# Downsampled attention scores: four half-array matmuls in two PSUM banks instead of three with a block-diagonal operand

## What is computed

```python
q_d = q.reshape(B, H, Sd, factor, D).mean(axis=3)     # Sd = 144, factor = 4, D = 64
k_d, v_d = ...                                        # the same
out_d = sm_attn(q_d, k_d, v_d)                        # 144 x 144 scores for each head
out_up = np.repeat(out_d, factor, axis=2)
...                                                   # local attention, |i - j| < 4
x = (out_up + out_local) as (B*S, H*D)
x = leaky_relu(x @ w_in1) @ w_out1                    # d_model 512, d_ff 2048
x = h - tanh(h), h = x @ w_in2; x @ w_out2
```

## Time and profile before

| what | value |
|---|---|
| median of three runs | 989.72 us (986.1 to 992.62) |
| the profiled execution, its own time | 990.84 us |
| its span, first to last instruction | 989.1 us |
| TensorE's granted clock, mean over the span | 0.984 of full speed |
| busy, share of the span | TensorE 97%, DVE 59%, ACT 56%, POOL 42% |

### The profile page before, as it was taken

How to read it: one execution, slowest core, us unless ns; L and a number is a source line. 1 busy time by engine, 2 the same in 40 slices (tenths; PEclk the granted TensorE clock), 3 DMA queues, 4 the chain that set the end, 5 groups by cost and what they waited for, 6 DMA issues and landing times.

```text
span 989.1 us, 19759 instructions
## 1 busy us (share of the span) xinstructions
PE 956.0 (97%) x6960; PEld 892.1 (90%) x6960; DVE 579.4 (59%) x1066; ACT 554.5 (56%) x1355; POOL 411.5 (42%) x341
## 2 busy tenths in 40 slices
PE   6789999999999999999999999999999999999998
PEld 5678999999999999999999988889899899898996
DVE  5745653664556446635324766776676676766764
ACT  4445644544635446446354767775575666766654
POOL 4535732723616417227161837623233233233232
PEclk9769999999999999999999999999999999999999
DMA  7842421022112211210100302100000000000000
GB/s 168 179 138 66 112 50 35 16 49 49 25 24 49 49 25 24 49 27 10 55 1 30 110 24 76 42 33 1 1 32 1 32 0 0 32 0 0 32 1 32
DMA packets 87797, 41.48 MB, mean 42 GB/s; under 512 B 60352, under 2 KB 81344, under 8 KB 87744
## 3 DMA queue, kind: packets, MB, share of 16 engines
q1 hardware_dynamic: 87744, 40.78, 15.7%
HBM read 36.04 MB, written 4.72 MB: 41 GB/s over the span
## 4 chain that ended last, share of the span: by engine, by line
PE 78%; ACT 6%; DVE 6%; POOL 5%; issue 3%; DMA 2%; SPq 0%; ACTq 0%; POOLq 0%; DVEq 0%
PE ph L474 12%; PE ph L476 11%; PE ph L475 11%; PE acc L550 6%; PE acc L551 6%; PE acc L552 6%; PE acc L503 6%; PE acc L504 5%; PE acc L505 5%; PE banks L372 3%; PE banks L404 2%; DVE g_lo L872 2%; POOL pl L993 2%; PE banks L391 2%; POOL g_lo L1039 1%
## 5 line engine op out<-in xcount | busy, mean ns | idle before, releaser
L1039 POOL TENSOR_TENSOR g_lo<-scratch,g_hi 128x384 fp32r<-128x384 f32 x96 | 126.1, 1314 | 259.3 <-ACT g_hi L664 259.3
L887 DVE TENSOR_TENSOR g<-g,ph 128x288 f32<-128x288 f32 x128 | 57.9, 452 | 189.4 <-ACT g L684 188.5
L1009 POOL TENSOR_TENSOR in_lo<-w_whole,in_hi 128x512 fp32r<-128x512 f32 x64 | 83.8, 1310 | 160.9 <-ACT in_hi L648 159.7
L474 PE MATMUL ph<-x_hi,w_hi_a 128*128 128x288 f32 (+1 forms) x448 | 144.7, 323 | 1.9 <-DVE x_lo L867 1.9
L684 ACT ACTIVATE g<-ph 128x288 f32<-128x288 f32 x128 | 52.5, 410 | 157.2 <-PE ph L476 155.8
L476 PE MATMUL ph<-x_hi,w_lo_a 128*128 128x288 f32 (+1 forms) x448 | 140.5, 314 | 0.0
L475 PE MATMUL ph<-x_lo,w_hi_a 128*128 128x288 f32 (+1 forms) x448 | 140.4, 313 | 0.0
L923 DVE SCALAR_TENSOR_TENSOR scratch<-scratch,ph 128x384 f32<-128x384 f32 x96 | 53.2, 554 | 112.9 <-ACT scratch L729 108.0
L1014 POOL TENSOR_TENSOR out_lo<-w_whole,out_hi 128x512 fp32r<-128x512 f32 x64 | 86.4, 1350 | 56.3 <-ACT out_hi L652 55.6
L728 ACT ACTIVATE scratch<-ph 128x384 f32<-128x384 f32 x96 | 46.8, 488 | 108.4 <-PE ph L476 106.8
L872 DVE TENSOR_TENSOR g_lo<-g,g_hi 128x288 fp32r<-128x288 f32 x128 | 88.6, 692 | 2.7 <-ACT g_hi L664 2.7
(11 more groups left out here) (162 smaller groups left out, 2688.8 us busy)
## 6 DMA issues: line engine op xcount, KB each, us to landing
out_dram<-o_stage SPq DMA_DIRECT2D x18, 256.0 KB, 2.0
w_whole<-in_moe_w_in_dram SPq DMA_DIRECT2D x16, 256.0 KB, 3.6
w_whole<-in_moe_w_out_dram SPq DMA_DIRECT2D x16, 256.0 KB, 4.4
qn<-in_q_dram SPq DMA_DIRECT2D x28, 144.0 KB
kn<-in_k_dram SPq DMA_DIRECT2D x28, 144.0 KB
v4n<-in_v_dram SPq DMA_DIRECT2D x28, 144.0 KB
vw<-in_v_dram SPq DMA_DIRECT2D x28, 122.5 KB
scratch<-in_moe_w_in_dram SPq DMA_DIRECT2D x8, 256.0 KB, 2.9
```

Of the source, the lines that this page charges most:

```text
L474: pe.matmul(bank, whi, x_hi[:, c, 0:width], start=(c == 0), stop=False)
L1009: pool.tensor_tensor(in_lo[:, f % 2, :], w_whole[:, f - KEPT, 0:DM], in_hi[:, f % 2, :].bitcast(F32), ALU.subtract).then_inc(in_lo_done, 1)
L1039: pool.tensor_tensor(g2_lo[:, f % 3, :], g2[:, f % 2, :], g2_hi[:, f % 3, :].bitcast(F32), ALU.subtract).then_inc(g_lo_done, 1)
```

## The change

The block-diagonal operand goes. q is summed into `qdT`, 144 columns with both heads in their own rows, by one DVE instruction. Step 6 has four matmuls instead of three: two groups of 72 queries for each of two heads, each on 64 rows of the array; head 0's scores go to bank 0, head 1's to bank 1. So step 6 waits for bank 1 as well, and step 11 waits for bank 0 (the exponentials) where it waited for bank 1. The coarse probabilities have 72 partitions and four groups of 144 instead of 96 partitions and three groups, in the maximum, the exponentials, the scaling and the turns. The order of the engines' lists is unchanged.

```diff
-    QT = 3
+    QT = 4
...
-                self.qd_diag, self.kdT = place("qd_diag", [P, NB, 2, QM]), place("kdT", [P, SD_])
+                self.qdT, self.kdT = place("qdT", [P, SD_]), place("kdT", [P, SD_])
...
             def values_d(s, bank):
-                probs = s.pdT.rearrange("p g (n h m) -> p g n h m", n=NB, h=2)
...
-                                         probs[:, g, :, h, :], start=(g == 0), stop=(g == 1))
+                                         s.pdT[:, g, h * SD_:(h + 1) * SD_], start=(g == 0), stop=(g == 1))
...
                 elif step == 6:
                     pe.wait_ge(s.means_done, 2 * i + 2)
                     pe.wait_ge(s.bank_free[0], uses0(i, 3))
-                    for t in range(QT):
-                        last = pe.matmul(s.banks[0:QP, 0, t * SD_:(t + 1) * SD_],
-                                         s.qd_diag[:, 3 * t:3 * t + 3, :, :].rearrange("p n h m -> p (n h m)"),
-                                         s.kdT[:, :], start=True, stop=True)
+                    pe.wait_ge(s.bank_free[1], uses1(i, 3))
+                    for t in range(QT // 2):
+                        for h in range(2):
+                            rows = slice(h * D, (h + 1) * D)
+                            last = pe.matmul(s.banks[0:QP, h, t * SD_:(t + 1) * SD_], s.qdT[rows, t * QP:(t + 1) * QP],
+                                             s.kdT[rows, :], start=True, stop=True)
                     last.then_inc(s.bank_full[0], 1)
                 elif step == 11:
                     pe.wait_ge(s.norm_l, i + 1)
-                    pe.wait_ge(s.bank_free[1], uses1(i, 3))
+                    pe.wait_ge(s.bank_free[0], uses0(i, 4))
...
                     for t in range(QT):
-                        last = act.activation(s.pd[:, t, :], s.banks[0:QP, 0, t * SD_:(t + 1) * SD_], ACT.Exp,
+                        h, at = divmod(t * SD_, 2 * SD_)
+                        last = act.activation(s.pd[:, t, :], s.banks[0:QP, h, at:at + SD_], ACT.Exp,
...
-                    for h in range(2):
-                        rows = slice(h * D, (h + 1) * D)
-                        last = dve.tensor_reduce(s.qd_diag[rows, :, h, :],
-                                                 s.qT[rows, :].rearrange("p (n m f) -> p n m f", n=NB, f=FACTOR),
-                                                 AX_X, ALU.add)
-                    last.then_inc(s.means_done, 1)
+                    dve.tensor_reduce(s.qdT[:, :], s.qT[:, :].rearrange("p (m f) -> p m f", f=FACTOR), AX_X, ALU.add)\
+                        .then_inc(s.means_done, 1)
...
-                    quarter = s.banks[0:QP, 0, 0:QT * SD_].rearrange("p (t k) -> p t k", t=QT)
-                    dve.tensor_reduce(s.mxd[:, :], quarter, AX_X, ALU.max, negate=True).then_inc(s.max_d, 1)
+                    quarter = s.banks[0:QP, 0:2, 0:2 * SD_].rearrange("p h (t k) -> p h t k", t=2)
+                    dve.tensor_reduce(s.mxd[:, :].rearrange("p (h t) -> p h t", h=2), quarter, AX_X, ALU.max,
+                                      negate=True).then_inc(s.max_d, 1)
...
-                dve.memset(s.qd_diag[:, :, :, :], 0.0)
```

More of the change, by code:

```diff
@@ L113, in two_scale_attention_and_feed_forward @@
         in_xT = {"pT": 0, "vd": 0, "kdT": 0, "up": 0, "qT": 1, "pd": 1, "mxl": 1, "mxd": 1, "rs": 1,
-                 "vw": 2, "qd_diag": 2, "v4n": 3, "pl": 3}
+                 "vw": 2, "qdT": 2, "v4n": 3, "pl": 3}
         taken = [S] * CD
```

## The result

| what | before | after |
|---|---|---|
| median of four runs each | 988.95 us (986.1 to 992.62) | 1001.19 us (998.72 to 1002.86) |
| ratio, 95% interval | | 1.011 (1.0082 to 1.0139) |
| the profiled execution, its own time | 990.84 us | 1002.86 us |
| its span | 989.1 us | 1001.1 us |
| mean granted clock | 0.984 | 0.988 |

The kernel before has one run more here than in the table ahead of the prediction. The forecast was +0.7% and within 1%; it came out at +1.1%, inside the range of 990.0 to 1002.5. The second stage went as forecast. The first stage did not: it lost 7.4 us in the profiled execution (the slowest of the four) and some 3 to 5 us by the timed runs, where 0.8 was forecast.

What follows compares the result with a forecast made beforehand. TensorE, busy 97% of the span, was taken as the bound. Second pairs 5.7, first pairs 0.1 and first stage 0.8 summed to +6.6 us: 996.3 us against 989.72, range 990 to 1002.5.

Steps and rivals of the forecast that it cites:

- The halves overlap: Step 6 on TensorE: matmuls on different row halves run fully side by side, last start 0.37 us after the first.
- The rival without overlap: Step 6: row halves run one after the other, last start 0.85 us after the first; 1001.8 us in all, chance 0.15.
- Entry: Change of array shape going into step 6: 0.23 us instead of 0.13, so +0.10 us a pair.
- Exit: From step 6's last record to the second matmul behind it: 0.45 us instead of 0.25, +0.20 us a pair.
- Net without a wait: Step 6 a pair: entry +0.10, block -0.24, exit +0.20, together +0.06 us; bound without overlap +0.54.
- D: TensorE's lateness after step 6 in second pairs: wait for bank 1 0.63, block -0.24, exit +0.20, together 0.59 us.
- Four exponentials: ACT's exponentials up to the weight split: 0.36 us more than three, 1.45 us in all.
- The rival that they swallow it: Second pairs: ACT and POOL catch up, only D's excess over the L391 stall counts, 0.17 us each; 991.5 us, chance 0.13.
- A second pair: L391 in the second stage's second pairs comes 0.95 us later: 0.59 plus 0.36; six pairs make 5.7 us.
- The rival "faster": DVE's halved L816 brings L829 forward, the wait vanishes and L391's stalls close: -5 us, 985 us; chance 0.04.
- The first stage. ... Together 0.8 us.: First stage: 0.7 us for exponentials on the chain, 0.1 us for step 6 of the first pair; together 0.8 us.
- The 0.7 for the exponentials: First stage, B pair: the fourth exponential stands before the copy L628 that TensorE needs, twice 0.36 us.

Runs made afterwards that it cites:

- e1_wait_only: The kernel before with only the new wait for bank 1 in front of step 6; 3.4 us slower in all.
- e2_exp4_only: The kernel before with a fourth exponential that repeats the last group into spare columns; 2.8 us slower in all.
- e4_filled: The changed kernel with three unused 128x128 matmuls ahead of step 6 of the first B pair; 998.26 us, ratio 1.0076 to the kernel before.
- f12_after_filled: The changed kernel with unused filler matmuls ahead of steps of the first stage and at its end; 996.08 us, ratio 1.0062 to the kernel before.
- f9: The changed kernel with bank 1 freed early on DVE and round 10's weight split listed ahead of the second pair's exponentials on ScalarE; 1012.74 us.

## Why the prediction was right, and where it was not

**Right, with sizes (forecast, measured):**
- The halves overlap. Last record's start 0.37, 0.43 us after the first; the two records of a pair of halves start 7 ns apart. The rival without overlap wanted 0.85: fell.
- Entry 0.23, 0.22 to 0.23. Exit from the last record to the second matmul behind 0.45, 254.23 - 253.78 = 0.45. Net without a wait +0.06, +0.11.
- The wait for L827 hits all second pairs and no first pair but the first stage's. D 0.59, 1.58 - 1.00 = 0.58. That the two agree so well is in part luck: step 6 started 0.05 us after L827's end and not 0.13, and its last record came 0.43 us after the first and not 0.37.
- Four exponentials 1.45, 1.44; L838 0.75, 0.75; no row of TensorE's waits in the changed kernel names POOL's longer scaling of `pd`.
- The stalls swallow nothing in second pairs: the one at L391 grew by 0.36 (0.26 to 0.62). The rival that they swallow it fell. It held for the wait alone: in `e1_wait_only` 0.24 was absorbed. In first pairs 0.10 went into the stall, as argued.
- A second pair +0.95, +1.0; six of them 5.7, 6.
- The halved L816 moved nothing: L827 still ends 0.65 us after L506 starts, where L829 ended 0.64 after L505. The rival "faster" fell, for the reason given, DVE's idle time behind it.

**The step that failed: "The first stage. ... Together 0.8 us."** It measured 7.4 us in the profiled execution. In the timed runs the whole difference is 9.1 to 10.9 us (0.0092 and 0.011 of 990); less 6 for the tiles, that leaves 3 to 5, or 4 to 6 if the 1.3 us that the profiles gain in the second layer stand in the timed runs too, which was not measured. The 0.7 for the exponentials was too high rather than too low: `e2_exp4_only` lost 0.36 us there. Two things were missed. First, the new wait was priced at step 6 of the first A pair alone, where it measured 0.46 us (13.81 against 13.35) for the 0.36 of the sum. At the B pairs it was put at nothing, without a reason. At the first of them the inversion of the A pair (L852, L854) stands between the sum of k and L827, and POOL holds it, so TensorE was 1.14 us more idle (1.42 against 0.28); at the second it stood 1.10 us, where the kernel before did not stand. Secondly, and much larger, the clock was taken as given. The sum used the lower clock for what step 6 itself costs and never asked what a longer stand does to the clock of the work behind it. The rows were there: the clock in that stage was not the full one, so its TensorE work could still take up to twice its time or come back from it. The Trainium skill, TensorE: Matmul & The Clock Gate, Part 1: The HAM clock gate, says that its clock is set by how busy it has been recently; `e4_filled`, in which three matmuls in the idle time changed the clock of the following 17 us, agrees, and `e1_wait_only` shows the same loss from a wait alone.

That the time still fell into the range is owed to the room left for the no-overlap rival, not to this mechanism: the upper end was right for the wrong reason.

**What stays open:** why one execution of a kernel is granted the higher clock in the first stage and another is not (there is one profile per kernel; `f12_after_filled` shows that fillers don't settle it), how much of the 3 to 5 us of the timed runs is the clock, since only the profiles divide them, and what turns the order of POOL and DVE round in `f9`.

## What to carry to other kernels

A new wait is priced by what stands ahead of the releaser in its engine's list at every place where it occurs, the start-up stage too, and there its price is not its length: where the granted clock is still moving, ask what TensorE's longer stand does to the work behind it, and read the clock from the durations of equal blocks. Matmuls that fill such a stand are tried on both kernels, or their gain is taken for the cure of a loss. Halving an engine's work that ends in idle time buys nothing, while a shape change of the array costs about 0.3 us in and out together (0.1 and 0.2) and eats what small overlapped blocks gain. A POOL chain without gaps can hold a DVE instruction for its whole length, so moving work ahead on POOL has to be checked against DVE's next two-operand instruction, not only against POOL's own due times.

## What the runs showed of the hardware that was not expected

- Row halves of full-precision matmuls that write the same columns in two PSUM banks run fully side by side: at 2.4 GHz the two of a pair start 7 ns apart, 0.12 us a slot (253.35 us of the changed kernel).
- A stand of TensorE 1.1 us longer at 21 us was followed by 30 us without 2.4 GHz; three small matmuls in that place gave 17 us of it. The same 36 records take 1.69 or 2.98 us.
- Within one kernel the timed executions are ordered by their mean granted clock: 987.64 us at 0.991, 995.34 at 0.977.
- A DVE instruction of 0.45 us took 4.95 behind four consecutive POOL instructions, and 0.45 where it came 0.02 us ahead of the first.
